# Attention, expert routing and a gated MLP in one kernel: residents' loads spread over the batches, scores last in a slot, growth table in parts, dummy matmuls in the first routing

## What is computed

```python
def _attn_ref(q, k, v):              # 4 batches, 8 heads, 768 steps, head size 64
    for t in range(S):
        state = gamma * state + outer(k[t], v[t])     # per batch and head
        y[t] = scale * q[t] @ state
def _moe_ref(x, w_gate, w1, w2):     # 3072 tokens, 512 wide, 8 experts, cap 384 each
    # all (token, expert) logits in falling order; a token goes to the first
    # expert that still has room; then per expert
    h = np.maximum(x[mask] @ w1[e], 0.0)
    out[mask] = h @ w2[e]
def _moe2_ref(x, w_gate, w_val, w_out):
    gate = 1.0 / (1.0 + np.exp(-(x @ w_gate)))
    return gate * (x @ w_val) @ w_out                 # 512 -> 1536 -> 512
```

## Time and profile before

| | us |
|---|---|
| median of three runs (lowest, highest) | 1080.89 (1080.59, 1082.13) |
| the profiled execution, its own time | 1084.76 |
| span of that execution, first to last instruction | 1082.7 |
| TensorE busy (share) | 1027.4 (95%) |
| VectorE busy (share) | 697.5 (64%) |
| ScalarE busy (share) | 330.0 (30%) |
| GpSimd busy (share) | 116.6 (11%) |
| mean clock granted to TensorE, of 1.00 | 0.974 |

### The profile page before, as it was taken

How to read it: one execution, slowest core, us unless ns; L and a number is a source line. 1 busy time by engine, 2 the same in 40 slices (tenths; PEclk the granted TensorE clock), 3 DMA queues, 4 the chain that set the end, 5 groups by cost and what they waited for, 6 DMA issues and landing times.

```text
span 1082.7 us, 20008 instructions
## 1 busy us (share of the span) xinstructions
PE 1027.4 (95%) x7130; PEld 958.4 (89%) x7130; DVE 697.5 (64%) x1880; ACT 330.0 (30%) x630; POOL 116.6 (11%) x141
## 2 busy tenths in 40 slices
PE   8999734999999999999999999999999999999996
PEld 7888623999999999999999999999999999999995
DVE  4777578777577657766776677666775677554211
ACT  3222423422333233322332333233412341234110
POOL 4212601033000101010100010011001100110001
PEclk9999865999999999999999999999999999999998
DMA  8899843403241324122322332132314231323000
GB/s 197 202 222 229 224 137 117 119 29 93 74 146 40 88 78 128 59 83 83 110 77 59 107 108 79 49 117 92 95 39 127 80 107 38 119 78 117 1 1 30
DMA packets 197356, 107.69 MB, mean 99 GB/s; under 512 B 81936, under 2 KB 182800, under 8 KB 197264
## 3 DMA queue, kind: packets, MB, share of 16 engines
q1 hardware_dynamic: 193424, 93.94, 31.2%
q0 software_dynamic: 3840, 12.59, 3.6%
HBM read 88.41 MB, written 18.09 MB: 98 GB/s over the span
## 4 chain that ended last, share of the span: by engine, by line
PE 93%; DVE 2%; DMA 1%; issue 1%; SPq 1%; ACT 0%; POOL 0%; DVEq 0%; POOLq 0%; ACTq 0%
PE bank L1323 21%; PE bank L1325 21%; PE bank L1324 21%; PE bank L1416 6%; PE bank L1417 6%; PE bank L1415 6%; PE bank L636 2%; PE bank L688 2%; PE bank L684 2%; PE bank L648 1%; PE bank L1277 1%; PE bank L655 1%; PE bank L698 1%; PE bank L668 1%; PE bank L610 1%
## 5 line engine op out<-in xcount | busy, mean ns | idle before, releaser
L1323 PE MATMUL bank<-h2h,resident 128*128 128x384 f32 x768 | 261.2, 340 | 0.0
L1325 PE MATMUL bank<-h2h,resident 128*128 128x384 f32 x768 | 257.9, 336 | 0.0
L1324 PE MATMUL bank<-h2l,resident 128*128 128x384 f32 x768 | 257.3, 335 | 0.0
L1323 PEld LDWEIGHTS bank<-h2h,resident 128*128 128x128 f32 x768 | 144.4, 188 | 2.9
L1324 PEld LDWEIGHTS bank<-h2l,resident 128*128 128x128 f32 x768 | 144.3, 188 | 2.9
L1325 PEld LDWEIGHTS bank<-h2h,resident 128*128 128x128 f32 x768 | 144.1, 188 | 0.0
L834 ACT ACTIVATE ring<-ring_raw 128x512 fp32r<-128x512 f32 x192 | 117.7, 624 | 61.7 <-DMA ring_raw<-in_moe_w_out_dram 42.0
L1150 DVE TENSOR_TENSOR pf<-bank,gate 128x384 f32<-128x384 f32 x96 | 53.5, 557 | 123.7 <-PE bank L1325 115.9
L858 ACT ACTIVATE ph<-pf 128x384 fp32r<-128x384 f32 x96 | 50.4, 525 | 252.1 <-DVE pf L1150 252.1
L1159 DVE TENSOR_TENSOR ring<-ring_raw,ring 128x512 fp32r<-128x512 f32 x192 | 126.0, 682 | 0.0
L854 ACT ACTIVATE gate<-bank 128x384 f32<-128x384 f32 x96 | 46.9, 489 | 145.9 <-PE bank L1325 145.8
(11 more groups left out here) (192 smaller groups left out, 1642.4 us busy)
## 6 DMA issues: line engine op xcount, KB each, us to landing
ring_raw<-in_moe_w_dram SPq DMA_DIRECT2D x128, 256.0 KB, 3.0
ring_raw<-in_moe_w_out_dram SPq DMA_DIRECT2D x64, 256.0 KB, 2.8
qraw<-in_q_dram SPq DMA_DIRECT2D x24, 256.0 KB, 3.3
kraw<-in_k_dram SPq DMA_DIRECT2D x24, 256.0 KB, 3.7
vraw<-in_v_dram SPq DMA_DIRECT2D x24, 256.0 KB, 4.2
xrows<-xrow SPq DMA_DIRECT2D x96, 64.0 KB, 2.3
xlaid<-xg SPq DMA_DIRECT2D x7, 768.0 KB, 4.4
zg<-xlaid SPq DMA_DIRECT2D x28, 192.0 KB, 4.2
```

The source lines that it names most:

```text
L1323: nc.tensor.matmul(ps, wh, xhi, start=start, stop=False)
L1324: nc.tensor.matmul(ps, wh, xlo, start=False, stop=False)
L1325: return nc.tensor.matmul(ps, wl, xhi, start=False, stop=stop)
```

## The change

Residents: EARLY goes from 16 to 8, two a batch, loaded in the passes s with s % 6 of 4 or 5; POOL makes both parts of them. Scores move to the end of TensorE's slot, and masking to the end of VectorE's. The growth table is made in six parts, three before the slots and three at the ends of slots 1 to 3. The partial logits get `ps_g` as a bank of their own. In the first routing `keep_busy` issues matmuls whose result nothing reads.

```diff
-        EARLY = 16
-        GROUPED = 4
+        GROUPED = 2
+        EARLY = GROUPED * B
@@ attend_sync, pass s
-                    if s >= U - C + 1 and group < EARLY // GROUPED:
-                        for r in range(group * GROUPED, (group + 1) * GROUPED):
-                            load_resident(sp, r)
-                        group += 1
+                    if s < U and s % C >= C - GROUPED:
+                        load_resident(sp, s // C * GROUPED + s % C - C + GROUPED)
@@ attend_gpsimd
+                def split_early(r):
+                    resident_landed(pool, r)
+                    nc.gpsimd.tensor_copy(resident[:, r, 0, :], resident_raw[r][:, :]).then_inc(early_hi, 1)
+                    pool.wait_ge(early_hi, r + 1)
+                    resident_low(r)
+
                 for b in range(B):
                     for c in range(C):
                         scale_k(b, c)
+                        if b > 0 and 0 < c <= GROUPED:
+                            split_early(GROUPED * (b - 1) + c - 1)
...
-                for r in range(EARLY):
-                    pool.wait_ge(resident_hi, r + 1)
-                    resident_low(r)
+                for r in range(EARLY - GROUPED, EARLY):
+                    split_early(r)
@@ attend_scalar: growth parts 0, 2 first, 4 in slot 2
-                        nc.scalar.activation(lparts[:, cc % 2, :], ps_l[:, P:2 * P], ACT.Copy).then_inc(parts_ready, 1)
-                    if s is not None and s >= U - C + 3:
-                        while highs[0] < min(EARLY, 3 * (s - U + C - 2)):
-                            high(act, highs[0])
-                            highs[0] += 1
+                        nc.scalar.activation(lparts[:, cc % 2, :], ps_g[:, 0:P], ACT.Copy).then_inc(parts_ready, 1)
@@ attend_vector: growth part 1 first, 3 and 5 in slots 1 and 3; masking (alive(s, 2)) behind xTa and state (alive(s, 3))
@@ attend_tensor: scores (alive(s, 2)) behind y and kv (alive(s, 3))
-                for c in range(C):
+                for c in range(3):
+                    turn_growth(c)
...
+                        if s is None or s - 5 >= 1:
+                            pe.wait_ge(logits_saved, u)
                         nc.tensor.matmul(ps_l[:, 0:E], lparts[:, cc % 2, :], pick[:, :], start=True, stop=True).then_inc(logits_done, 1)
...
                         if s is None or s - 4 >= 1:
-                            pe.wait_ge(logits_saved, u)
+                            pe.wait_ge(parts_ready, u)
...
+                    if s in (1, 2, 3):
+                        turn_growth(s + 2)
@@ gpsimd, late residents
             for r in range(EARLY, RESIDENT):
                 pool.wait_ge(val_done if r % 2 else gate_done, (r - EARLY) // 2 + 1)
-                low(r)
+                late_low(r)
@@ tensor, first routing
+            def keep_busy(times):
+
+                for n in range(times):
+                    nc.tensor.matmul(PS_OUT[0][:, 0:NF], ones[:, :], segment[:, :, :].rearrange("p e u -> p (e u)"), start=True, stop=True)
+
             def transpose_x():
                 for j in range(TT):
+                    if j > 0:
+                        keep_busy(8)
                     pe.wait_ge(third_gathered[j], 16)
...
+            keep_busy(36)
             for vis in range(VISITS):
                 visit(vis, 0)
+                if vis < V_TIE - 1:
+                    keep_busy(10)
+                elif vis < V_IDS:
+                    keep_busy(20)
+                else:
+                    keep_busy(60)
             transpose_x()
```

More of the change, by code:

```diff
@@ L348, in retention_moe_glu_kernel, with slots @@
             xrow_stored = [sem(f"xrow_stored{c}") for c in range(C)]
-            def slots(eng, body, first, last, unrolled=1):
+            def slots(eng, body, first, last):
                 s = first
@@ L356, in slots @@
                     s += 1
-                looped = B + 1 - unrolled
-                with eng.Fori(1, looped) as b:
+                with eng.Fori(1, B) as b:
                     for c in range(C):
                         body(b, c, None)
-                for s in range(looped * C, last + 1):
-                    body(s // C, s % C, s)
+                for s in range(U, last + 1):
+                    body(B, s - U, s)
             def unit(b, c, lag):
@@ L503, in attend_scalar, with scale_growth @@
                     act.sem_inc(xrow_stored[c], STORED)
-                for c in range(0, C, 2):
+                def scale_growth(c):
                     act.wait_ge(growth_turned, c + 1)
@@ L530, in body, with scale_growth @@
                             act.wait_ge(logits_done, u - 1)
-                        nc.scalar.activation(lparts[:, cc % 2, :], ps_l[:, P:2 * P], ACT.Copy).then_inc(parts_ready, 1)
-                    if s is not None and s >= U - C + 3:
-                        while highs[0] < min(EARLY, 3 * (s - U + C - 2)):
-                            high(act, highs[0])
-                            highs[0] += 1
-                slots(act, body, 0, U + 3, unrolled=2)
-                assert highs[0] == EARLY
+                        nc.scalar.activation(lparts[:, cc % 2, :], ps_g[:, 0:P], ACT.Copy).then_inc(parts_ready, 1)
+                slots(act, body, 0, U + 3)
             def attend_vector(dve):
                 nc.vector.memset(state[:, :, :, :], 0.0).then_inc(state_cleared, 1)
-                for c in range(1, C, 2):
+                def scale_growth(c):
                     dve.wait_ge(growth_turned, c + 1)
@@ L564, in body @@
                                             xTa[:, cc % 2, :, :].rearrange("p a (t i) -> p a t i", i=QUAD)).then_inc(xrow_ready, 1)
[L565 to L574, removed]
                     if alive(s, 3):
@@ L599, in body @@
                                 ins.then_inc(state_ready, 1)
+                    if alive(s, 2):
+                        bb, cc = unit(b, c, 2)
+                        u = bb * C + cc
+                        for half in range(2):
+                            dve.wait_ge(scores_done, 2 * u + half + 1)
+                            if half == 0 and (s is None or s - 2 >= 2):
+                                dve.wait_ge(y_done, u - 1)
+                            nc.vector.tensor_tensor(
+                                att[:, cc % 2, half:H:2, :], ps_s[half][:, :].rearrange("p (a t) -> p a t", a=NPAIR),
+                                causal[:, :].unsqueeze(1).to_broadcast([P, NPAIR, P]), ALU.mult).then_inc(att_ready, 1)
+                    if s in (1, 3):
+                        scale_growth(s + 2)
                 slots(dve, body, 0, U + 4)
@@ L622, in body @@
                             pe.wait_ge(pick_made, 1 + KD)
+                            pe.wait_ge(growth_odd, 3)
+                        if s is None or s - 5 >= 1:
+                            pe.wait_ge(logits_saved, u)
                         nc.tensor.matmul(ps_l[:, 0:E], lparts[:, cc % 2, :], pick[:, :], start=True, stop=True).then_inc(logits_done, 1)
[L624 to L639, removed]
                     if alive(s, 1):
@@ L664, in body @@
                             pe.wait_ge(wr_loaded, 16)
+                            pe.wait_ge(growth_even, 3)
                         if s is None or s - 4 >= 1:
-                            pe.wait_ge(logits_saved, u)
+                            pe.wait_ge(parts_ready, u)
                         for a in range(KD):
-                            last = nc.tensor.matmul(ps_l[a * GROUP:(a + 1) * GROUP, P:2 * P], wr[:, a, :], xTa[:, cc % 2, a, :],
+                            last = nc.tensor.matmul(ps_g[a * GROUP:(a + 1) * GROUP, 0:P], wr[:, a, :], xTa[:, cc % 2, a, :],
                                                     start=True, stop=True)
@@ L701, in body @@
                             last.then_inc(kv_done, 1)
+                    if alive(s, 2):
+                        bb, cc = unit(b, c, 2)
+                        u = bb * C + cc
+                        pe.wait_ge(kT_ready, u + 1)
+                        if s == 2:
+                            pe.wait_ge(growth_even, 1)
+                            pe.wait_ge(growth_odd, 1)
+                        if s is None or s - 2 >= 1:
+                            pe.wait_ge(att_ready, 2 * u)
+                        for a in range(NPAIR):
+                            for half in range(2):
+                                rows = slice(half * D, half * D + D)
+                                last = nc.tensor.matmul(ps_s[half][:, a * P:(a + 1) * P], kT[rows, cc % 2, a, :],
+                                                        qT[rows, cc % 3, a, :], start=True, stop=True)
+                                if a == NPAIR - 1:
+                                    last.then_inc(scores_done, 1)
+                    if s in (1, 2, 3):
+                        turn_growth(s + 2)
                 slots(pe, body, 0, U + 4)
@@ L792, in gather, with late_low @@
```

(7 more changed lines are left out.)

27 lines of the change are left out of this document (17 added, 10 removed).

## The result

| | kernel before | kernel after |
|---|---|---|
| median | 1080.74 us (4 runs, 1078.68 to 1082.13) | 1099.43 us (4 runs, 1098.80 to 1100.19) |
| ratio to before | 1 | 1.0171, 95% interval 1.0155 to 1.0188 |
| profiled execution (span, mean clock) | 1084.76 us (1082.7, 0.974) | 1100.19 us (1098.5, 0.983) |

The change costs 18.7 us by the medians and 15.4 by the profiled executions. Forecast were 1094 in the median's terms and 1098.0 in the profiled execution's. The gap between the two readings lies in before: its profiled execution stood 4 us above its median, that of after 0.8.

What follows compares the result with a forecast made beforehand. TensorE bounds attention and everything after 186 us, VectorE's small instructions the first routing. +2.9 - 4.3 + 14.6 = +13.2 gives 1098.0 us profiled, 1094 us in the median's terms; range 1084 to 1101.

Steps and rivals of the forecast that it cites:

- +2.9: Attention, net: ScalarE's wait for residents removed, -7.5 us, against TensorE's new wait for ks, +10.4 us.
- Round 0, +14.6: Round 0: POOL's late splits hold gather(1), turning 14 us late; TensorE idles 12.4 us, plus 2.2 for its clock.
- the price that was put on one fall of the clock: Any stall where TensorE's clock falls to half: about 2.2 us lost before it is back.
- Rival C: Round 0: gather(1) isn't held or its lateness is absorbed, so not slower: 1079.5 us, with A about 1070; chance 0.06.
- ks behind the residents, +10.4: Attention, slot 9: POOL waits for late resident loads before ks of unit 8; later slots 15 and 21 add almost nothing.
- Rival A: Attention: SP's lateness does not reach TensorE, -7.5 + 1.2 instead of +2.9: 1085 us; chance 0.16.
- ScalarE's wait, -7.5: Attention: ScalarE's wait for residents goes, 5.34 us of idle TensorE plus 2.2 for the clock.
- The dummies, -4.3: First routing: dummies keep the clock up; digits, folds and later matmuls gain 2.6 us, first products 1.7, transposes nothing.
- rival B: First routing: the dummies do not hold the clock, so the -4.3 is gone: 1102 us; chance 0.12.
- Order and bank, 0: Attention: scores last and the partial logits' change; middle slots unchanged, last slots nothing within 1.3 us either way.
- the +1.2: Attention's head: new order delays the start by 1.2 us; covered by slot 9's wait, so nothing in the sum.
- The late residents: First routing: twenty late residents instead of twelve; eight more loads and copies cost nothing, without cover up to 8 us.

Runs made afterwards that it cites:

- the one with the late gather: Kernel before with only the late splits' waits moved to product (r - EARLY) // 2 + 5, holding gather(1): 1094.66 us, ratio 1.0116.
- the one with the bank: Kernel before with only a bank of its own for the partial logits and the waits that go with it: 1080.32 us, ratio 0.9998.
- the repaired versions: After with gather(1) between splits, POOL's early splits later in the batch, no dummies: 1076.58 us; another chip 1075.71; with one run of 96 dummies 1075.71.
- gather between the splits: Kernel after with gather(1) put between the late splits of r = 21 and r = 22, the splits' waits unchanged: 1085.88 us, ratio 1.0039.

## Why the prediction was right or wrong

**The sign and the place were right.** 1099.43 lies inside the range, 5.4 us above the point. The main mechanism, read from POOL's order and in no line of the diff's own, showed step by step. In the profiled execution's terms the forecast came within 2.2 us (1098.0, measured 1100.19), and that is partly luck: the traces put +1.2, +1.6 and +12.9 where it had +2.9, -4.3 and +14.6, so the dummies missed by 5.9 and the other two by 3.4 the other way.

**Round 0, +14.6: right, slightly high.** The stall is 10.7 us instead of 12.4 idle. The forecast's own figures, 14.0 late less 1.8 of slack, give 12.2, so 0.2 of the miss is its arithmetic. Landing of the lay-out took 3.7 us instead of 4.4, quartering 5.2 instead of 6.0. The rest of the 12.9, 2.2 us, is the price that was put on one fall of the clock. Measured alone on before it costs 12.9, taken from after 13.6. Rival C is out.

**ks behind the residents, +10.4: right in its place, a bit high in size.** Ready at 49.23 instead of 51.6: the resident landed 1.8 us sooner than summed, and the copy on POOL takes 0.61 us, not 1.04. Slot 10 is 7.75 us late. That slots 15 and 21 add almost nothing was right: 1.43 and 0.27. Undone, it gives 9.7. Rival A is out.

**ScalarE's wait, -7.5: true of the profiled execution, too large for the median.** This step fails in the median's terms. In the trace the attention ends 1.2 us later than before, for +2.9 forecast. But the stall was read from one execution, and then the 3.9 us by which that execution stood above the median came off the total. Two more kernels have before's residents and its order in the attention: the one with the late gather, and the one with the bank. In their profiles the last logits come at 136.4 and 133.0 instead of 138.8. The wait is 2.4 and 1.4 us, and the two slots around it are 4.0 and 2.1 us longer than two of 5.15, where before's are 7.5 longer. These two executions stood 0.7 above and 1.6 below their medians. So the excess sat, by all that these runs show, in the very stall that the change removes, and goes with it: at the median the stall was worth some 4 us (an estimate, 7.5 less 3.9), and after's profile stands only 0.8 above its own median. With the excess left on the stall the same sum gives 1098 in both terms. That one stall holds the whole excess is argued from these three profiles, not shown by a run of its own.

**The dummies, -4.3: wrong, sign included.** Three steps failed. The 2.6 us for digits and folds took a price from products of 128 columns; these matmuls take 0.51 us at 1.00 and 0.53 at 0.50, so a digit's 2.4 us did not shrink. The transposes were booked at nothing with dummies of 0.08 us; in after's profile the clock had fallen before them, and the sixteen took 3.0 us, so that transposes to first product took 6.0 instead of 3.5 (5.3, 5.5 and 4.0 in the three other profiles with these dummies). Last, the rows of the first gather come later with the dummies of after: gather to transposes is 5.9 to 6.6 us in five kernels, against 5.0 to 5.4 in six without any, 1.2 us more in after. What delays it stays open: after's trace has two instruction transfers on one queue between 150 and 186 us where before's has one, and nothing was tried on it. The gain on the first products did come, 1.8 us for 1.7. In after's trace it makes +3.4 - 1.8 = +1.6, by the medians 2.7. The clock was held through most of the routing, so rival B's reason was only half right, though its 1102 was nearer than the point.

**Order and bank, 0: missed a gain.** The forecast asked nothing of the middle slots; they are 0.1 us shorter, some 2 us in the whole attention. The head did not move: slot 5 starts at 22.51, before at 22.52, so the +1.2 needs no cover. In the last slots the waits are 0.8, 0.8 and 0.5 us where before has 1.7 in two: 0.4 more, within the 1.3 allowed. The late residents, booked at nothing, cost nothing that shows: TensorE's waits name no load of theirs.

**The balance by medians.** 13.6 + 9.7 + 2.7 = 26.0 for the three losses, less about 4 and 2, gives +20, measured +18.7; the repaired versions, where the three are gone, should then gain 6 and gain 4.3 to 5.2. By medians it closes within 1 to 2 us. By the ratios to before, each on its own chip, it closes less well. The three losses are then 14.3, 11.6 and 4.2 us, 30 in all against the 18.5 of after, and the repaired kernel should gain some 11 to 12 us where it gains 5 to 6. Taken together the intervals of these ratios leave about 6 us open (an estimate). So each loss is shown and placed, but a few us of overlap between them, the rival of the repaired kernel, are not ruled out.

## What to carry to other kernels

A constant that moves work from one stage to another also moves every wait that is counted from it: look for what is queued behind that wait on an in-order engine, in loops the diff leaves alone. Before a stall's removal is booked, see whether the profiled execution stands above the median; the excess may lie in the very stall, and then it comes off the stall and not off the total. Dummy matmuls can pay only where the work behind them is bound by the clock. Here that was the transposes and the first products, and no run here made them pay: with the dummies of after the rows came later, and with 96 in one row they outlasted the landing.

## What the hardware showed unexpectedly

- Six matmuls of 32 columns in bf16 take 0.51 us at a granted clock of 1.00 and 0.53 at 0.50.
- POOL's back-to-back subtractions of 128x512 lengthen VectorE's instructions with two SBUF inputs from 0.56 to 1.60 us and from 0.17 to 1.26; its instruction with one input in PSUM stays at 0.56.
- A 128x512 copy to fp32r takes POOL 0.61 us, a subtraction of that size 1.26.
- TensorE's clock fell in one wait of 3.20 us (after) and stayed at 1.00 in one of 3.21 us (gather between the splits), behind the same sixty dummies.
